# Token blocks of the expert layers and the feed-forward: loaded by feature quarters and turned in 32x32 squares by VectorE, with the seam between the two phases laid anew

## The reference

```python
# 1. a decaying linear attention, batch 4, heads 8, sequence 768, head size 48
S_re, S_im = decay * S + k v^T ;  y[t] = q[t] @ S_re
x = y as [3072 tokens, 384 features]
# 2. eight experts, one for each token
e = argmax(x @ w_gate);  gate = softmax(x @ w_gate)[e] * sigmoid(x @ w_output_gate)[e]
x = gate * (relu(x @ w1[e]) @ w2[e])            # w1 384x1024, w2 1024x384
# 3. a feed-forward for all tokens
h = x @ w_in;  out = max(0.01 * h, h) @ w_out   # w_in 384x2048, w_out 2048x384
```

## Time and profile before

| | |
|---|---|
| median of three runs | 1002.3 us |
| the profiled execution: its time, its span | 1002.58 us, 1000.6 us |
| attention, up to the first token load | 0 to 294.9 us |
| experts | 294.9 to 586.0 us |
| feed-forward | 586.0 to 1000.6 us |
| busy over the span: PE, VectorE, ScalarE, GpSimd | 95%, 41%, 45%, 51% |
| mean granted TensorE clock | 0.987 |

### The profile page before, as it was taken

The page is one execution under the profiler, slowest core; times in us unless marked ns, Lnnn a source line. Parts: engine busy times, 40 slices in busy tenths (PEclk is TensorE's granted clock), DMA queues, the critical chain, the costliest instruction groups (busy, mean ns, idle before and its releaser), DMA issues.

```text
span 1000.6 us, 17624 instructions
## 1 busy us (share of the span) xinstructions
PE 949.9 (95%) x5980; PEld 846.0 (85%) x5981; DVE 412.9 (41%) x742; ACT 454.2 (45%) x772; POOL 509.5 (51%) x429
## 2 busy tenths in 40 slices
PE   6999999999839999999999999999999999999997
PEld 5778788888727999998998989999999999999996
DVE  6889988988824323333232322212112122112111
ACT  7999889996612222222222333333333333333322
POOL 4235665665547558568839943243343332433433
PEclk9999999999968999999999999999999999999999
DMA  4643454320342343253535520010010010000000
GB/s 145 174 136 104 148 171 130 118 81 28 100 169 95 109 166 120 85 167 115 154 106 165 189 57 17 16 40 16 9 40 17 24 32 17 32 1 1 32 1 32
DMA packets 47192, 84.06 MB, mean 84 GB/s; under 512 B 23813, under 2 KB 36377, under 8 KB 44569
## 3 DMA queue, kind: packets, MB, share of 16 engines
q1 hardware_dynamic: 40984, 48.59, 16.3%
q0 software_dynamic: 6144, 34.65, 9.9%
HBM read 65.80 MB, written 17.38 MB: 83 GB/s over the span
## 4 chain that ended last, share of the span: by engine, by line
PE 74%; ACT 10%; DVE 5%; issue 5%; POOL 5%; SPq 1%; DMA 1%; POOLq 0%; DVEq 0%; ACTq 0%
PE bank L2127 20%; PE bank L2140 20%; PE bank L2085 11%; PE bank L2107 10%; POOL wm L1866 3%; PE bank L2095 2%; PE bank L1096 2%; DVE neglog L848 1%; PE bank L1178 1%; PE bank L1136 1%; POOL wm L1864 1%; PE bank L1164 1%; PE bank L1138 1%; PE bank L1106 1%; PE bank L1119 1%
## 5 line engine op out<-in xcount | busy, mean ns | idle before, releaser
L1894 POOL TENSOR_TENSOR act_r<-act_f,act_r 128x512 fp32r<-128x512 f32 x96 | 124.6, 1298 | 260.3 <-ACT act_r L1955 257.6
L2140 PE MATMUL bank<-w_out_r,act_r 128*128 128x384 f32 x1152 | 217.7, 337 | 0.3 <-POOL act_r L1894 0.3
L2127 PE MATMUL bank<-x,w_in_r 128*128 128x512 f32 x864 | 216.7, 395 | 0.0
L2140 PEld LDWEIGHTS bank<-w_out_r,act_r 128*128 128x128 f32 x1152 | 204.8, 188 | 8.8 <-POOL act_r L1894 0.6
L2016 DVE TENSOR_TENSOR act_f<-bank,small 128x512 f32<-128x512 f32 x96 | 66.5, 693 | 292.7 <-ACT small L1952 275.2
L2127 PEld LDWEIGHTS bank<-x,w_in_r 128*128 128x128 f32 x864 | 159.6, 188 | 29.5
L1952 ACT ACTIVATE small<-bank 128x512 f32<-128x512 f32 x96 | 57.5, 599 | 191.2 <-PE bank L2127 191.1
L2085 PE MATMUL bank<-wm,x_tr 128*128 (+1 forms) x522 | 129.5, 402 | 4.0 <-POOL wm L1866 1.7
L2107 PE MATMUL bank<-wm,h_tr 128*128 (+1 forms) x696 | 128.6, 339 | 0.7 <-DVE h_tr L2000 0.7
L2107 PEld LDWEIGHTS bank<-wm,h_tr 128*128 128x128 f32 x696 | 120.1, 188 | 0.9 <-issue 0.9
L2085 PEld LDWEIGHTS bank<-wm,x_tr 128*128 128x128 f32 x522 | 97.8, 192 | 25.1 <-issue 5.0
(11 more groups left out here) (195 smaller groups left out, 1406.4 us busy)
## 6 DMA issues: line engine op xcount, KB each, us to landing
stage<-moe_w POOLq DMA_DIRECT2D x12, 1536.0 KB, 7.0
qkv_in<-in_qkv SPq DMA_DIRECT2D x24, 576.0 KB, 6.0
a_in<-in_a SPq DMA_DIRECT2D x11, 768.0 KB, 5.1
stage<-moe_w SPq DMA_DIRECT2D x4, 1536.0 KB
x_b<-x_sorted SPq DMA_DIRECT2D x30, 193.0 KB
y_sorted<-y_b SPq DMA_DIRECT2D x29, 192.0 KB
xg<-y_sorted SPq DMA_DIRECT2D x24, 192.0 KB, 2.4
stage<-w_out POOLq DMA_DIRECT2D x2, 1536.0 KB, 7.3
```

Of the source, the lines that this page charges most:

```text
L1894: pool.tensor_tensor(a[:, 1, :], act_f[f % 2][:, :], a[:, 0, :].bitcast(F32), ALU.subtract).then_inc(s_gl, 1)
L2127: last = pe.matmul(h_bank[f % 2][:, :], w_in_r[:, wp, t * F2 + f * P:t * F2 + (f + 1) * P], window_part(w, xp)[:, t, :], start=(t == 0 and ...
L2140: last = pe.matmul(o_bank[j][:, 0:W], a[:, ap, j * P:(j + 1) * P], w_out_r[:, wp, f * W:(f + 1) * W], start=(f == 0 and n == 0), stop=(f = ...
```

## The change

Token tiles are no longer transposed by TensorE. SP loads a tile of 128 rows in four DMAs, one for each quarter of the features: quarter a (96 features) goes to partitions 32a to 32a+31, and there the 128 tokens lie as four groups of 32. One VectorE `transpose` then turns all 32x32 squares of the 128x384 tile into a PSUM bank, which leaves features on partitions in a new order (`by_quarter`); w1 and w_in are laid out in that order on the host. `transpose_block`, `transpose_token` and `gated` are gone. The gates come by a small DMA of their own (`gates`, 128 elements of 4 bytes) and are multiplied in by `relu`'s scale.

The waits for expert weights become finer: GpSimd's w1 half waits for the layer 1 of expert e-2's last block, its w2 half for that block's layer 2; `layer1` waits for the w1 half alone (`ready`), `layer2` for both.

At the seam, the loops end one block earlier, and the last two blocks are written out. `layer2` of the next to last block is cut in the middle by `transpose_hidden` of the last. The tiles of window 0 are loaded as soon as twelve blocks are stored, and turned by VectorE between the last two blocks' work. The feed-forward's `h_bank` becomes banks 5 and 6, tiles are turned in bank 4 alone, and the last result has bank 7. SP now has 16 DMAs for the tiles of window 1 ahead of the one for `ids`.

The core of the diff:

```diff
-        def load(g):
-            sp.dma_start(x_b[:, :], xs[rows, :]).then_inc(s_xb, 16)
+        def load(g):
+            need(sp, s_tx, g)
+            rows = rows_of(g)
+            for a in range(Q):
+                sp.dma_start(x_q[a * SQ:(a + 1) * SQ, :].rearrange("i (b c) -> i b c", b=Q),
+                             quarters(xs[rows, 0:W], a)).then_inc(s_xb, 16)
+        def gates(g):
+            need(sp, s_h, 2 * g)
+            sp.dma_start(gate_b[:, :], xs[rows_of(g), W:W + 1], allow_slow_non_contiguous=True).then_inc(s_gate_in, 16)
...
         sp.wait_ge(s_rows, 1)
-        sp.wait_ge(s_tx, 1)
         load(1)
+        load(2)
+        gates(1)
...
-        with sp.Fori(1, before) as g:
-            sp.wait_ge(s_tx, g + 3)
+        with sp.Fori(1, third) as g:
             load(g + 3)
+            gates(g + 2)
             store(g)
-        sp.wait_ge(s_ys, before * 16)
-        window(0)
-        store(before)
-        store(last_g)
-        sp.wait_ge(s_ys, last_g * 16 + 16)
-        window(1)
+        sp.wait_ge(s_ys, 16 * (TW + E))
+        for t in range(2):
+            tile_in(t)
+        gates(third + 2)
+        for t in range(2, TW):
+            tile_in(t)
+        store(third)
+        store(third + 1)
+        store(third + 2)
+        sp.wait_ge(s_ys, third * 16 + 48)
+        for t in range(TW, 2 * TW):
+            tile_in(t)
         sp.wait_ge(s_sorted, 16 * NCH)
         sp.dma_start(ids[:, :].unsqueeze(2), ...).then_inc(s_ids, 16)
...
-            if i == 0 and done is not None:
-                pool.wait_ge(s_p2, done)
+            if done is not None:
+                pool.wait_ge((s_p1, s_p2)[i], done)
...
+        def turn_tokens(g):
+            dve.wait_ge(s_xb, 64 * g + 64)
+            need(dve, s_xl, g)
+            dve.transpose(tx_bank[:, 0:W].rearrange("p (k b i) -> p b k i", b=Q, i=SQ),
+                          x_q[:, :].rearrange("p (b k j) -> p b k j", b=Q, j=SQ)).then_inc(s_tx, 1)
...
         dve.tensor_copy(table[:, 0:TB], tf[:, 0:TB]).then_inc(s_rows, 1)
+        turn_tokens(0)
         block_tokens(0)
+        turn_tokens(1)
...
-        with dve.Fori(1, before) as g:
+        with dve.Fori(1, third) as g:
             trailing(g)
             block_tokens(g + 2)
+            turn_tokens(g + 3)
             result(g)
...
-            if layer == 1:
-                pe.wait_ge(s_wh, at(pe, T_READY, g, 2, 2 * E))
+            ready = at(pe, T_READY, g, 1, 2 * E - 1)
+            pe.wait_ge(s_wh, ready if layer == 1 else ready + 1)
...
-        with pe.Fori(1, last_g) as g:
+        with pe.Fori(1, third + 1) as g:
             transpose_hidden(g)
             layer1(g + 1)
-            transpose_block(g + 2)
             layer2(g)
-        for j in range(2):
-            transpose_token(0, j)
-        transpose_hidden(last_g)
-        for j in range(2, TW):
-            transpose_token(0, j)
-        layer2(last_g)
+        transpose_hidden(third + 1)
+        layer1(third + 2)
+        layer2(third + 1, amid=third + 2)
+        layer2(third + 2, last_ye_bank)
```

More of the change, by code:

```diff
@@ L26 @@
 KT = W // P
+Q = 4
+SQ = P // Q
 FT1 = F1 // P
@@ L1643, in route, with route_vector @@
     s_d = sem("route_vector_step")
-    def route_vector(dve, block_tokens):
+    def route_vector(dve, turn_tokens, block_tokens):
         count = [0]
@@ L1966, in body @@
             flush(w)
-        gated(0)
+        relu(0)
         act.wait_ge(s_table, 1)
         act.sem_inc(s_use, 4)
[L1971 to L1974, removed]
+        third = second_before_last(act)
+        with act.Fori(0, third + 1) as g:
             leading(g)
-            gated(g + 2)
             relu(g + 1)
+        leading(third + 1)
         for j in range(2):
             tokens(0, j)
-        leading(last_g)
+        relu(third + 2)
         for j in range(2, TW):
             tokens(0, j)
+        leading(third + 2, third + 2)
+        act.wait_ge(s_p2, third + 3)
         for f in range(2):
@@ L2020, in body @@
                 hidden(FT2 * w + f, f)
+                if f - 1 in AT and more:
+                    turn(w + 1, AT[f - 1])
                 if f - 2 in AT and more:
@@ L2025, in body @@
                     hidden(FT2 * (w + 1) + f, f)
-        route_vector(dve, block_tokens)
+        route_vector(dve, turn_tokens, block_tokens)
         sorted_slots(dve)
@@ L2032, in layers_vector @@
         dve.sem_inc(s_o, TW)
-        last_g = last_block(dve)
-        before = at(dve, T_LAST, 1, N // P - 2, NBMAX - 2)
+        third = second_before_last(dve)
         block_tokens(1)
+        turn_tokens(2)
         trailing(0)
         block_tokens(2)
+        turn_tokens(3)
         result(0)
-        with dve.Fori(1, before) as g:
+        with dve.Fori(1, third) as g:
             trailing(g)
             block_tokens(g + 2)
+            turn_tokens(g + 3)
             result(g)
-        trailing(before)
-        block_tokens(before + 2)
-        result(before)
-        for j in range(2):
-            tokens(0, j)
-        trailing(last_g)
-        for j in range(2, TW):
-            tokens(0, j)
-        result(last_g)
+        trailing(third)
+        block_tokens(third + 2)
+        result(third)
+        trailing(third + 1)
+        dve.wait_ge(s_xl, third + 3)
+        for j in range(0, TW, 2):
+            turn(0, j)
+            turn(0, j + 1)
+            tokens(0, j)
+            tokens(0, j + 1)
+        trailing(third + 2, (0,))
+        result(third + 1)
+        trailing(third + 2, (1,))
+        result(third + 2, last_ye_bank)
         for f in range(2):
@@ L2056, in layers_tensor @@
     def layers_tensor(pe):
-        def transpose_block(g):
-            pe.wait_ge(s_xg, g + 1)
-            need(pe, s_xl, g)
-            for j in range(KT):
-                last = pe.transpose(tx_bank[:, j * P:(j + 1) * P], x_b[:, j * P:(j + 1) * P], ident[:, :])
-            last.then_inc(s_tx, 1)
         def part_of(base, at_col, n):
@@ L2110, in layer2 @@
             last.then_inc(s_p2, 1)
-        def transpose_token(w, j):
-            t = TW * w + j
-            pe.wait_ge(s_in[j], 16 * (w + 1))
-            need(pe, s_tl, t - 1)
-            for k in range(KT):
-                last = pe.transpose(tt_bank[j % 2][:, k * P:(k + 1) * P], xg[j][:, k * P:(k + 1) * P], ident[:, :])
-            last.then_inc(s_tt, 1)
         def ff1(w, f):
@@ L2155, in body @@
                     ff2(w, f)
-                if f in AT and more:
-                    transpose_token(w + 1, AT[f])
             if not more:
```

103 lines of the change are left out of this document (60 added, 43 removed).

## The result

The changed kernel takes 991.88 us in the median of four runs (989.56 to 993.04), beside 1002.73 for the kernel before in the runs that go with them. The ratio is 0.9888, with a 95% interval of 0.9865 to 0.9910: faster by 1.1%, which is 11.2 us of 1002.3, where 16.8 had been forecast. Carried to the 1002.3 of the blind text the ratio gives 991.1, just inside the upper end of the range of 982.5 to 991.5. The profiled execution took 991.69 us, its span is 989.9, so it stands for the median.

The account below looks back on a forecast made before the run. TensorE, busy 99.13 of 100 us, was taken as the bound. Terms +1.6 - 9.2 - 2.2 - 2.7 + 2.3 - 6.6 = -16.8 from 1002.58 gave 985.8, stated as 985.5 us; range 982.5 to 991.5.

Parts of the forecast that it names:

- The token transposes: Removed from TensorE's path: 28 x 0.33 = 9.2 us off among the experts, 20 x 0.33 = 6.6 in the feed-forward.
- What VectorE gets: VectorE's turn of a block: 0.56 us, at most 2.8; hidden unless a turn takes 2.9 us.
- the loop as a mechanism: Result, store, one-buffer load, landing, turn: 4.28 us plus landing, 6.84 in all, under the block of 9.19.
- so it costs nothing: The claim that VectorE's turn and its load loop, 6.84 us, stay hidden under the new block of 9.19.
- the case of a weight load beside it: Load-loop rival: landings of 6.0 us beside GpSimd's weight loads make the loop the bound, about 1020 us; chance 0.05.
- signs of being wrong: Blocks over 9.19, landings above 4.9 us, clock of 0.50 behind 308, VectorE turns of several microseconds, seam waits for h_tr.
- Small packets: Block loads in 384-byte packets: lower bound nothing added, taken; upper 1.9 us a load. Slow-packets rival: 992.2 us, chance 0.13.
- The start: Layer 1 of block 1 starts at 311.7 in place of 310.12, since the table comes later: +1.6 us.
- The clock rival: At the start, the clock rises only after the pause; layer 1 of block 1 takes 7.07: +2.7, 988.2 us; chance 0.10.
- Expert boundaries: Finer weight waits remove 1.1 us lost at each of two boundaries behind experts of three blocks: 2.2 off.
- The seam: Between layer 2 of block 27 and ff1, 7.72 us become 5.06: 2.7 off.
- The token numbers: Twelve more DMAs ahead of ids, 5.3 us against 3.0 of slack, delay ff2(0, 2): +2.3 us.

Follow-up runs that it names:

- a4: Against the changed kernel, VectorE turns block 1 behind the table's steps, not ahead of them: 988.1 us, ratio 0.9823 to the kernel before.
- b3: Against the changed kernel, three spare TensorE transposes of a constant in each place of the removed ones: 1005.25 us, ratio 1.0011 to the kernel before.
- e2: Against the changed kernel, TensorE reads the table's weight count once a block; layer 1 waits for both halves: 988.46 us, ratio 0.9854.
- d2: Against the kernel with earlier block loads, later block 1 turn and earlier token numbers, x_tr's start aligned to 32 bytes: 983.98 us, ratio 0.9808.

## Why the prediction was right in kind and short in size

- **The token transposes.** Right: 0.33 us for three among the experts and 0.35 in the feed-forward, by the spare ones. What bounded the kernel was read rightly from the chain.
- **What VectorE gets.** The duration was right (0.594 for 0.56), and so was the loop as a mechanism: result, store, load, landing, turn. *The step that failed is the one behind it*, "so it costs nothing", by two terms. The landing was taken from one load that had the engines to itself, 2.56 from issue to use; the case of a weight load beside it got a chance of 0.05 as a cause for a slower kernel and no price inside a faster one. Beside a weight load the landing is 4 to 7.6 us behind the last issue, at nine blocks of the profile after. And the rest of the loop was added up to 4.28, where the chain has 5.65: from the end of the store's issue to the first quarter's it is 1.50 us (0.74 written down), from the first quarter's issue to the last's 1.80 (1.33). So the loop binds from a landing of 3.6 us, not of 4.9. One late load is within VectorE's slack: landings of 7.0 to 7.3 us behind an on-time load (block 11 in the profile after and in a4) cost 0.25 us at most. TensorE stopped where two came in a row, 4.5 or 4.6 and then 7.4 or 7.6 us, and 1.8 to 3.6 us were lost, the larger figure with the lower clock behind it. Two of the signs of being wrong were there, a landing above 4.9 us and a clock of 0.50 behind 308 (at 364 to 368). The earlier load takes the wait away.
- **Small packets.** The lower bound was the right choice.
- **The start.** +1.4 for +1.6, by the steps written down. The clock rival was given 0.10. A slow layer 1 of block 1 came in seven of the ten profiles that had the pause, at 1.4 to 2.6 us, so its chance was far too low. Its course was another: the clock always rose within the first layer 1, and in those seven it fell back in or just behind the pauses. In the three profiles with the late turn, whose pauses are 0.84 to 0.94 us, it did not fall. The Trainium skill (TensorE: Matmul & The Clock Gate, Part 1) describes a clock that follows recent activity, and these profiles agree with it, with 0.58 to 1.00 within the first layer 1 and 0.50 behind the pauses: 7.0 us against 4.46 for the same 18 matmuls.
- **Expert boundaries.** Right, 2.2 before; undone in the new kernel it costs 3.3.
- **The seam.** Right: 7.72 to 5.04, of which the cut is 1.9.
- **The token numbers.** The term was +2.3. The wait was 2.1 to 2.2 in two profiles, and the lower clock behind it added up to 1.8.
- **Layer 1.** 4.21 in place of 4.13 in every block. With a layer 2 of 4.17 for 4.19 the block is 0.06 longer than forecast, 1.6 us over the loop. I had no term for it. Neither transposes between the layers (b3) nor the table read (e2) nor the start of x_tr (d2) make it. The cause stays open.

Together: among the blocks 5.4 us missed, of which 3.6 are the two late loads with the clock behind them, 1.6 the longer block and 0.2 block 11's load; in the feed-forward 1.2, which is 1.8 of clock less 0.4 that the transposes gave above their price and 0.2 by which the wait was shorter.

That the time still fell inside the range is in part luck. The upper end of the range stood at 991.5 for the sake of slow packets, which did not come; what came in their place had no price.

## What to carry to other kernels

Where an engine of 95% busy time hands work to one that is busy for a third of it, the gain is read well from the chain of waits, and what can spoil it is the order in the queues that now carry more: here a load behind a store, a turn ahead of a table, and 12 more DMAs ahead of one on which another engine waits. A landing time is to be taken from the busiest moment that the trace shows, beside the transfers that will be in flight, not from the load that had the engines alone. A loop through several queues is to be added up from every gap in them, loop jumps and address reads too, and asked what two late landings in a row do. And a pause of TensorE of 2 us must be given two prices, its own and that of the matmuls behind it at the lower clock.

## What the runs showed of the hardware that had not been expected

- After pauses of TensorE of 1.6 to 2.3 us the granted clock fell to the lower level in some profiles (24 matmuls in 6.00 us, 12 in 3.40, 18 in 7.00) and stayed at the upper one in others (24 in 4.44, 12 in 2.37). The same code gave both. Even at the upper level the first group behind a pause took 0.25 to 0.29 us more than in a stream (4.44 for 4.17, 4.46 for 4.21, 2.37 for 2.08).
- A quarter load of 384-byte pieces and a load of whole 1536-byte rows land equally late beside a weight load of 1.5 MB and a run of indirect DMAs (5.7 to 7.6 and 5.9 to 6.4 us after the last issue, at blocks 7, 11, 15 and 19, the one load with slow issues left out) and equally soon without them (1.4 to 1.7 and 1.4 to 1.5).
- A fp32 VectorE transpose of 128x384 values from SBUF to PSUM, in 32x32 squares and with a reordered output, takes 0.594 us, 0.04 more than a copy of the same size out of PSUM.
